# The hand-written turn of the fourth routed slot, the order of two weight loads, and the first slot's splits in a fused recurrence, dense layer and mixture of experts

## What is computed

```
x  = mLSTM recurrence over (batch 4, heads 8, 768 steps, head size 40)   -> [3072, 320]
x  = act(x @ w_in) @ w_out          # w_in [320, 2048], w_out [2048, 320]
logits = x @ w_gate                 # 8 experts
e  = argmax(logits);  gate = softmax(logits)[e]
out = gate * (relu(x @ w1[e]) @ w2[e])   # w1 [8, 320, 1024], w2 [8, 1024, 320]
```

## Time and profile before

| | us |
|---|---|
| median of 3 runs | 823.09 (822.97 to 824.31) |
| the profiled execution | 822.7 |
| its span (first to last instruction) | 820.8 |
| TensorE busy | 764.8 (93%) |
| VectorE, ScalarE, GpSimd busy | 593.6, 423.7, 322.6 |
| mean granted TensorE clock, share of full | 0.987 |

### The profile page before, as it was taken

The page is one execution under the profiler, slowest core; times in us unless marked ns, Lnnn a source line. Parts: engine busy times, 40 slices in busy tenths (PEclk is TensorE's granted clock), DMA queues, the critical chain, the costliest instruction groups (busy, mean ns, idle before and its releaser), DMA issues. The chain is left out here.

```text
span 820.8 us, 17200 instructions
## 1 busy us (share of the span) xinstructions
PE 764.8 (93%) x5765; PEld 743.4 (91%) x5765; DVE 593.6 (72%) x1006; ACT 423.7 (52%) x649; POOL 322.6 (39%) x297
## 2 busy tenths in 40 slices
PE   2788999999999999999999999999849999999994
PEld 1788999999999999999999999989849999999994
DVE  4653868787878787887878888668647676867850
ACT  3023445454545454545455455646645676757751
POOL 3352543534343545444454534550723323232111
PEclk9999999999999999999999999999988999999998
DMA  7962232222222322232233200544887535545300
GB/s 213 301 166 75 77 91 76 91 75 91 74 91 77 95 83 94 88 95 83 92 92 96 78 16 1 183 117 97 264 308 238 184 109 192 164 151 169 116 20 5
DMA packets 41458, 97.05 MB, mean 118 GB/s; under 512 B 6936, under 2 KB 24482, under 8 KB 39755
## 3 DMA queue, kind: packets, MB, share of 16 engines
q1 hardware_dynamic: 37498, 87.46, 34.1%
q0 software_dynamic: 3920, 9.08, 3.9%
HBM read 105.63 MB, written 9.33 MB: 140 GB/s over the span
## 5 line engine op out<-in xcount | busy, mean ns | idle before, releaser
L545 POOL TENSOR_TENSOR g_t<-u_t,r_t 128x512 f32<-128x512 f32 x96 | 135.9, 1416 | 254.6 <-ACT u_t L695 254.5
L690 ACT ACTIVATE r_t<-bank,neg 128x512 f32<-128x512 f32 x96 | 66.0, 688 | 186.6 <-PE bank L1388 186.6
L1400 PE MATMUL bank<-wo_h,g_h 128*128 128x328 f32 x384 | 127.2, 331 | 0.0
L1002 DVE TENSOR_SCALAR u_t<-bank 128x512 f32<-128x512 f32 x96 | 66.1, 689 | 75.3 <-ACT r_t L690 47.5
L1400 PE MATMUL bank<-wo_h,g_l 128*128 128x328 f32 x384 | 120.1, 313 | 0.0
L1400 PE MATMUL bank<-wo_l,g_h 128*128 128x328 f32 x384 | 120.1, 313 | 0.0
L627 POOL DMA_INDIRECT out_x<-ob,idx_tok x31 | 39.2, 1264 | 157.6 <-ACT ob L765 153.3
L695 ACT ACTIVATE u_t<-u_t,half 128x512 f32<-128x512 f32 x96 | 69.4, 723 | 40.6 <-DVE u_t L1002 38.7
L938 DVE TENSOR_TENSOR_SCAN W<-W,cst 128x512 f32<-128x512 f32 x48 | 83.2, 1737 | 4.4 <-DMA W<-decays 4.4
L1521 PE MATMUL bank<-w_h,h_h 128*128 128x320 f32 x248 | 79.1, 319 | 3.7 <-DVE w_l L1063 2.6
L1388 PE MATMUL bank<-xT_h,wi_h 128*128 (+1 forms) x384 | 78.8, 287 | 1.6 <-issue 1.6
(11 more groups left out here) (231 smaller groups left out, 1947.1 us busy)
## 6 DMA issues: line engine op xcount, KB each, us to landing
raw<-in_w SPq DMA_DIRECT2D x12, 1280.0 KB
W<-decays SPq DMA_DIRECT2D x24, 512.0 KB, 5.3
raw<-in_w SPq DMA_DIRECT2D x12, 1024.0 KB
raw2n<-in_w SPq DMA_DIRECT2D x7, 1280.0 KB
raw1n<-in_w SPq DMA_DIRECT2D x7, 1024.0 KB
raw<-in_w SPq DMA_DIRECT2D x24, 256.0 KB
qG<-in_q SPq DMA_DIRECT2D x24, 180.0 KB
qT<-in_qt SPq DMA_DIRECT2D x48, 80.0 KB
```

Source lines behind the costliest of these rows:

```text
L545: pool.tensor_tensor(g_t[p % 2][:, :], u_t[p % 2][:, :], r_t[p % 2][:, :], ALU.add).then_inc(sm["g_done"], 1)
L690: act.activation(r_t[p % 2][:, :], bank_h[p % 2][:, :], ACT.Relu, bias=neg1[:, 0:1]).then_inc(sm["r_done"], 1)
L1002: dve.tensor_scalar(u_t[p % 2][:, :], bank_h[p % 2][:, :], 1.0, -1.0, ALU.min, ALU.max).then_inc(sm["u_done"], 1)
L1400: mm = pe.matmul(bank_acc[tt][:, 0:DL], l[p % 4][:, c], r[:, f, :], start=f == 0 and a == 0, stop=f == NT1 - 1 and a == 2)
```

## The change

It reorders instructions and adds none. `route_expert` is cut in two, its first two instructions now being `route_top`.

- ScalarE and VectorE: the order of slots 2 to 4 is changed and written by hand up to slot 5's w1 splits, and the loop begins at slot 4 instead of 3. The splits of slot 5's w1, which stood ahead of the evictions of slots 3 and 4, now stand behind all of them.
- SP: from `load_routed2(3)` on the order was refill(3), refill(4), refill2(2), refill2(3), and is refill2(2), refill(4), refill(3), refill2(3).
- Last dense block: the two halves of slot 0's w1 are split at steps 3 and 5 on ScalarE and 4 and 5 on VectorE, where it was step 5 and the block's tail. The tail is reordered: `w2_high(0, 0)` ahead of `g_high`, `h_low(0, 0)` and `h_low(0, 1)` further up on VectorE, and on TensorE `first_wide(0, 2)` ahead of `rank`.

```diff
@@ SP @@
             load_routed2(3)
+            refill2(2)
+            refill(4)
             refill(3)
-            refill(4)
-            refill2(2)
             refill2(3)
@@ ScalarE, body and tail @@
-                    if not att and p == 5:
-                        w1_high(0, 0)
+                    if not att and p in (3, 5):
+                        w1_high(0, p // 4)
...
             def tail(t):
-                w1_high(0, 1)
+                w2_high(0, 0)
                 g_high(t, NP1 - 1)
-                w2_high(0, 0)
                 x2_copy(t, 0)
@@ ScalarE, slots 2 to 5 @@
             h_high(2, 2)
+            w2_high(2, 1)
+            h_high(2, 3)
             w1_high(3, 0)
-            h_high(2, 3)
-            w2_high(2, 1)
+            y_high(3)
             w1_high(3, 1)
             w1_high(4, 0)
-            y_high(3)
             w1_high(4, 1)
+            act.wait_ge(sm["list_done"], 2)
+            h_plain(3, 0)
+            h_plain(3, 1)
+            y_high(4)
             w2_high(3, 0)
+            out_gate(2)
+            hT_high(3, 0)
+            hT_high(3, 1)
             w2_high(3, 1)
-            act.wait_ge(sm["list_done"], 2)
-            for s in range(EARLY, NS):
+            h_high(4, 0)
+            w2_high(4, 0)
+            h_high(4, 1)
+            w2_high(4, 1)
+            h_high(4, 2)
+            h_high(4, 3)
+            w1_high(5, 0)
+            w1_high(5, 1)
+            for s in range(EARLY + 1, NS):
@@ VectorE, body and tail @@
                     if prev and p == 3:
+                        route_top(t - 1)
                         route_expert(t - 1)
...
-                        if p == 5:
-                            w1_low(0, 0)
+                        if p in (4, 5):
+                            w1_low(0, p - 4)
...
             def tail(t):
                 g_low(t, NP1 - 1)
-                w1_low(0, 1)
+                route_top(t)
+                h_low(0, 0)
                 route_expert(t)
-                h_low(0, 0)
+                h_low(0, 1)
                 route_gate(t, True)
                 route_slot(t)
...
-            h_low(0, 1)
             w2_low(0, 0)
@@ VectorE, slots 2 to 5: the low steps @@
             h_low(2, 2)
+            w2_low(2, 1)
+            h_low(2, 3)
             w1_low(3, 0)
-            h_low(2, 3)
-            w2_low(2, 1)
+            y_low(3)
             w1_low(3, 1)
             w1_low(4, 0)
-            y_low(3)
             w1_low(4, 1)
+            y_low(4)
             w2_low(3, 0)
+            hT_low(3, 0)
+            hT_low(3, 1)
             w2_low(3, 1)
-            for s in range(EARLY, NS):
+            h_low(4, 0)
+            w2_low(4, 0)
+            h_low(4, 1)
+            w2_low(4, 1)
+            h_low(4, 2)
+            h_low(4, 3)
+            w1_low(5, 0)
+            w1_low(5, 1)
+            for s in range(EARLY + 1, NS):
@@ TensorE, tail @@
                 first_wide(0, 1)
+                first_wide(0, 2)
                 rank(t)
-                for p in range(2, 4):
-                    first_wide(0, p)
+                first_wide(0, 3)
```

More of the change, by code:

```diff
@@ L1016, in route_step, with route_top @@
                 dve.wait_ge(sm["route_step"], t * 9 + k)
-            def route_expert(t):
+            def route_top(t):
                 dve.wait_ge(sm["x2_ready"], t * 2 + 3)
@@ L1023, in route_expert @@
                 dve.tensor_tensor(sh[:, :, :], logit, mx[:, :].unsqueeze(2).to_broadcast([P, 2, E]), ALU.subtract).then_inc(sm["sh_ready"], 1)
+            def route_expert(t):
                 route_step(t, 2, dve.tensor_tensor(oh[:, :, :], logit, mx[:, :].unsqueeze(2).to_broadcast([P, 2, E]), ALU.is_equal))
```

## The result

The changed kernel takes 827.33 us (median of 20 runs, 824.43 to 832.25) against 824.27 us (20 runs, 822.37 to 826.16): a ratio of 1.0043, 95% interval 1.0027 to 1.0059. I had forecast 819.0 us and a 77% chance of faster; it is slower, the outcome that I gave 6%. The profiled execution took 825.41 us, with a span 2.7 us longer than that of before.

What follows compares the result with a forecast made beforehand. TensorE, busy 93% of 820.8 us, was held bound by waits of 10.5 and 2.6 us and the slow clock behind them. From 822.7 us, -2.5 (slots) and -1.6 (first slot) gave 818.6, as median 819.0; range 812 to 823.

Steps and rivals of the forecast that it cites:

- where the stall goes: Slot 5: its w2 load, queued behind slot 7's w1, keeps TensorE idle 5 to 8 us before first_wide(5,3).
- the clock: Behind the new stall at first_wide(5,3): TensorE comes back at half clock, costing +1.6 to +2.6 us, taken as +2.5.
- the 2.6 us wait: TensorE's wait for slot 2's w2 split: goes with its slow stretch once w2_high(2,1) runs right behind h_high(2,2).
- the slots' times: Slots 3 to 5: slot 5's w2 issued at 616.9 us, landed at 624.0, first_wide(5,3) at 627.5 against 632.47, -5.0 us.
- When L2(5) lands: Slot 5's w2 load: issued at 616.9 us, transfers from 615.4 at 342 GB/s, landing taken as 624.0.
- my third rival: Slower: slot 9's w1 load served beside slot 5's w2, landing 628.7 to 631.5 us; 823.7 to 826.5 us in all; chance 0.08.
- my lower bound of 5.8: Slot 5's w2 load: 5.8 us from issue to landing, from the old trace, so landing at 622.7 us.
- My upper bound, 10.1 us: Slot 5's w2 load: 10.1 us from issue, as slot 5's w1 took, so landing at 626.9 us.
- the first slot, -1.6 us: Slot 0's early splits and reordered tail: cost 0.6 us, waits removed up to 2.7, bounds 0 and -3, net -1.6.
- hardly moves: Slot 1's w2 load, issued behind w2_low(0,1), keeps its time and can give back most of the first-slot gain in slot 1.

Runs made afterwards that it cites:

- The swap: Changed kernel with slot 5's w2 load, refill2(4), issued ahead of slot 7's w1 load, refill(5), on SP: 816.14 us, ratio 0.9909 to the kernel before.
- the evictions first: Changed kernel with slot 5's four evictions ahead of its w2 splits on ScalarE and VectorE, loads unchanged: 814.12 us, ratio 0.9906 to the kernel before.
- the change with the wait ahead of the loop: Changed kernel plus one already satisfied wait on SyncE ahead of its last refill loop, no order changed: ratio 0.9997 to the kernel before.
- the wait at the end: Changed kernel plus one already satisfied wait on SyncE behind its last refill, no order changed: ratio 1.0016 to the kernel before.
- the change with L(9) held back: Changed kernel with slot 9's w1 load held until slot 5's first w2 split is made: 823.37 us, ratio 1.0009 to the kernel before.
- The pair with and without L(9): Changed kernel without its first-slot part, as such and with slot 9's w1 load held until slot 5's first w2 split: 822.28 us (0.9994) and 820.81 (0.9986).
- the part alone: Kernel before with only the early splits of slot 0's w1 and the reordered tail of the last dense block: 824.26 us against 822.72, ratio 1.0017.

## Why the prediction was wrong, by its steps

**Right: where the stall goes.** "refill(5) waits for both w1_low(5) ... and L2(5) can only follow it"; "the stall moves one slot on". ScalarE idle in front of slot 5's w2 split, TensorE idle in front of the last quarter of first_wide(5) at 632.65, one wait of 2.4 us at first_wide(5,0) (forecast 2 to 3), 1.07 at first_wide(4,2) (forecast 1.2), L2(5) issued 3.75 us behind L(7) (forecast 3.5). The swap and the evictions first take the stall away by two roads.

**Right: the clock.** +2.5 us forecast for the new stall, 2.5 measured from first_wide(5,3) to the end.

**Right for one build only: the 2.6 us wait.** It was read as an effect of the order of the splits. It goes with a wait added on SyncE alone, so most of it came from TensorE's late signals; the sum had no term for it.

**Right in size, in a build without the unnamed wait: the slots' times.** Times from the first gather of the routed list (577.53 before, 580.44 in the change with the wait ahead of the loop) shift by 2.91 us. On the clock of before, that kernel issues L(7) at 613.1 (forecast 613.3) and L2(5) at 616.9 (616.9), reads it at 624.75 (624.0) and starts first_wide(5,3) at 631.11 - 2.91 = 628.2 (627.5). The read was forecast 0.75 us too early, the issues within 0.2. With the wait at the end (first gather at 581.47, a shift of 3.94) the issues are at 613.0 and 617.15, and the read is at 626.8.

**The step that failed first: "When L2(5) lands", 7.1 us after an issue at 616.9.** In the kernel measured ScalarE reads it 10.2 us after an issue at 619.04: 629.2, past all the bounds I had set for the forecast (626.9), and past the 628.1 from which my third rival decides. Two things are in it. The issue is 2.1 us late because the unnamed wait delays slot 2's evictions, VectorE behind them and so w1_low(5) (to 613.76, forecast 611.8). And the load takes longer: no profile has it in 7.1 us. With the loads in the order of the change it is 7.7, 7.8, 7.9, 9.6, 9.8 (the evictions first) and 12.2 us (the slowest execution of the change with L(9) held back) in the six profiles without the unnamed wait, and 10.2, 10.5 and 9.3 in the three with it; the groups overlap. Even with the order of before, and the added wait, it is 8.0 (620.49 to 628.48, with ScalarE waiting), where my lower bound of 5.8 took the end of the transfers for the moment of use.

On the clock of before, counted from the first gather, the issue is at 616.6 to 617.3 and the read at 624.8 to 628.9 in those six, and at 619.0 to 620.3 and 629.2 to 629.8 in the three. The late issue goes with the unnamed wait; the time from issue to read does not clearly.

I had the queue start empty at 615.4, and it nearly was: ScalarE waits until 615.19 for slot 6's w1, issued from 602.61, with slot 6's w2 behind it, but from 597.93 to 615.29 the queue moved 4.29 MB of the 4.46 MB of slot 5's w1 and slot 6's two loads. So what was left ahead of L(7), some 0.2 MB, explains under 1 us of the 3.1. My upper bound, 10.1 us, was the nearer row; why is not settled.

**The rival that came true in size, not in mechanism.** 823.7 to 826.5 us was the slower case (0.08), with L(9) served beside L2(5). The pair with and without L(9) gives the same read to 0.05 us, so this mechanism does not hold there, and the 12.2 us were measured with nothing behind the load. That the size came out is luck: 2.1 us of it are a late issue that no rival had.

**The term with the wrong sign: the first slot, -1.6 us.** Alone the part is +0.17%, 1.4 us. From the issue of L(0) to the first gather of the routed list it takes 62.0 to 63.2 us, mean 62.5, in the nine profiles with the splits at their old steps, and 63.0 to 65.7, mean 64.3, in the eight with the early ones: 1.8 us more. I had the cost at 0.6, with a bound of 3.4. ScalarE's wait for L(0) is 2.2 us in the change and 3.0 with the part alone; relu_part(4) comes 8.70 us behind the issue of L(0) for 7.15 before, 1.6 us late where I had forecast 1.4, but the slack behind it that was to hide most of this was not there. What it was to give back came in the main (counted from L(0)'s issue, L(1) goes out 7.0 us sooner, forecast 9: 535.23 - 514.50 for 543.23 - 515.52; and the 5.87 us wait is gone). But L2(1), which "hardly moves", goes out 2.6 us later by the same count (555.39 for 553.81), and ScalarE waits for it, 1.4 us in the change and 2.6 with the part alone.

**The sum, closed on the profiled pair.** Forecast were -5.0 for the start of first_wide(5,3), +2.5 for the clock and -1.6 for the first slot, -4.1 in all. Measured are +0.2, +2.5 and 0, which is the 2.7 us between the spans. The first slot's cost does not show in this pair: the first gather is at 577.54 for 577.53, because L(0) happened to go out 1.0 us sooner (514.50 for 515.52). So of the 6.8 us between forecast and measurement 5.2 are in the step of L2(5) and 1.6 in the first slot's term. Of the 5.2, 0.8 to 4.9 are there without the unnamed wait too; the rest goes with the build, which was not in the sum at all.

**What stays open.** Why TensorE's signals come late in some builds. The profile calls the wait "remote", another core or an unknown queue, on a program of one core. In some of these profiles TensorE ("issue" waits of 1.1 us) and SyncE (the issue of slot 4's w2 at 582.60, lasting 0.69) are late at the same moment. Late instructions would fit, but the rows speak against them: of the two queues that the profile names "instruction", no packet moves between 579.22 and 588.53 us in the changed kernel, and none in the longest unnamed wait of the other four profiles. Why an added wait on SyncE removes it was not tried by itself. Nor is it settled why the load takes from 7.7 to 12.2 us in one order. For the first-slot part, 0.17% is smaller than what a build can shift, so I lean on its wait rows and on the two groups above, not on that ratio.

## What to carry to other kernels

When a load is pulled ahead of its old moment of need, look up which loads stand ahead of it in the queue and what each of those waits for; a free buffer is worth nothing behind a refill that waits for a later split. Put evictions, which free TensorE's banks, ahead of splits that wait for a load. And before a difference of under half a per cent is given to an order of work, build the same order once more with one idle wait added: here that alone moved it by as much. The same holds for a wait that an edit is to remove: the 2.6 us one was gone from the old order with an idle wait added.

## What the runs showed of the hardware

A wait that changes no order, added to a queue that isn't the bound, moved the time of three of the four builds by 0.27 to 0.53% (of the kernel before by nothing measurable) and took away waits of 1.0 to 4.4 us on another engine. Behind these waits is a semaphore of TensorE's that rose 3.0 to 6.7 us after the last matmul of its block, in five of 17 profiles, and within 0.1 us in the others. The same 1.3 MB load took from 7.7 to 12.2 us from issue to use with the loads in the order of the change, for reasons that are open, and 11.7 and 13.6 us when it was issued into a queue already holding slot 6's loads. And a stall costs by where it stands as well: the 0.54 clock behind first_wide(5,3) cost 2.4 us in 28 matmuls, nearly a third of the 8.15 us stall itself.
